# The last up-projection product of two tiles on the upper and lower 64 rows of TensorE, and the second network in pairs of tiles

## What is computed

```python
# 1: causal mixing over 7 tokens, weights = softmax of weight_gen per head (8 heads of 24)
out = einsum("bshk,bskhg->bshg", softmax(weight_gen), windows_of_7(x))
# 2: gated network, d_ff 1536
xn = x / sqrt(mean(x * x) + 1e-6) * rms_g
y = (silu(xn @ w_gate) * (xn @ w_val)) @ w_out
# 3: second network, d_ff 2048
h = y @ w_in
out = (h * sigmoid(1.702 * h)) @ w_out2
```

## Time and profile before

| | |
|---|---|
| three runs, median (lowest, highest) | 1329.49 us (1329.16 to 1329.7) |
| profiled execution, span from first to last instruction | 1328.2 us |
| PE busy, share of the span | 1283.0 us, 97% |
| PE weight loads | 1088.3 us, 82% |
| DVE busy | 782.2 us, 59% |
| ACT busy | 679.0 us, 51% |
| POOL busy | 101.7 us, 8% |

### The profile page before, as it was taken

The page is one execution under the profiler, slowest core; times in us unless marked ns, Lnnn a source line. Parts: engine busy times, 40 slices in busy tenths (PEclk is TensorE's granted clock), DMA queues, the critical chain, the costliest instruction groups (busy, mean ns, idle before and its releaser), DMA issues.

```text
span 1328.2 us, 19585 instructions
## 1 busy us (share of the span) xinstructions
PE 1283.0 (97%) x6304; PEld 1088.3 (82%) x6304; DVE 782.2 (59%) x1186; ACT 679.0 (51%) x1194; POOL 101.7 (8%) x104
## 2 busy tenths in 40 slices
PE   0889999999999999999999999999999999999998
PEld 0667888889888888888889888888888889888898
DVE  5889475473846638475473846638475473843432
ACT  2343646555464553646555454553645555464454
POOL 6873000000000000000000000000000000000000
PEclk9999999999999999999999999999999999999999
DMA  5331000000100001000000100001000000000000
GB/s 141 87 108 39 1 16 31 16 31 4 41 0 15 30 3 41 0 15 30 15 30 3 41 0 15 30 3 41 0 15 30 15 30 0 12 0 13 1 13 13
DMA packets 14525, 32.21 MB, mean 24 GB/s; under 512 B 1828, under 2 KB 7842, under 8 KB 14496
## 3 DMA queue, kind: packets, MB, share of 16 engines
q1 hardware_dynamic: 14496, 31.85, 7.6%
HBM read 25.55 MB, written 6.29 MB: 24 GB/s over the span
## 4 chain that ended last, share of the span: by engine, by line
PE 92%; DVE 1%; issue 1%; ACT 0%; DVEq 0%
PE acc L754 15%; PE up_ps L706 11%; PE up_ps L713 11%; PE up_ps L714 11%; PE up_ps L707 11%; PE up_ps L710 11%; PE acc L755 7%; PE acc L734 3%; PE acc L731 3%; PE acc L735 3%; PE acc L732 3%; PE acc L733 3%; PE acc L768 0%; DVE hidden L654 0%; PE acc L772 0%
## 5 line engine op out<-in xcount | busy, mean ns | idle before, releaser
L669 DVE TENSOR_TENSOR h_lo<-hidden,h_hi 128x512 fp32r<-128x512 f32 x448 | 315.7, 706 | 382.0 <-ACT h_hi L487 381.5
L487 ACT CAST h_hi<-hidden 128x512 fp32r<-128x512 f32 x448 | 278.7, 622 | 186.1 <-DVE hidden L654 178.5
L754 PE MATMUL acc<-out_w,h_hi 128*128 128x384 f32 x1024 | 306.4, 355 | 0.0
L755 PE MATMUL acc<-out_w,h_lo 128*128 128x192 f32 x1024 | 257.6, 252 | 0.0
L471 ACT ACTIVATE hidden<-up_ps 128x512 f32<-128x512 f32 x256 | 153.2, 598 | 203.2 <-PE up_ps L714 202.9
L466 ACT ACTIVATE silu<-up_ps 128x512 f32<-128x512 f32 x192 | 114.5, 596 | 196.1 <-PE up_ps L714 195.7
L654 DVE TENSOR_TENSOR hidden<-silu,up_ps 128x512 f32<-128x512 f32 x192 | 131.8, 687 | 129.0 <-ACT silu L466 128.8
L755 PEld LDWEIGHTS acc<-out_w,h_lo 128*128 128x128 f32 x1024 | 195.0, 190 | 10.2
L754 PEld LDWEIGHTS acc<-out_w,h_hi 128*128 128x128 f32 x1024 | 192.2, 188 | 10.6
L706 PE MATMUL up_ps<-x_hi,up_w 128*128 128x512 f32 x384 | 154.5, 402 | 3.1 <-DVE hidden L654 2.0
L713 PE MATMUL up_ps<-x_rest,up_w 128*128 128x512 f32 x384 | 152.7, 398 | 3.8 <-DVE x_rest L593 3.8
(11 more groups left out here) (80 smaller groups left out, 1671.1 us busy)
## 6 DMA issues: line engine op xcount, KB each, us to landing
x_win<-in_x_dram SPq DMA_DIRECT2D x14, 960.0 KB
out_dram<-out_sb SPq DMA_DIRECT2D x15, 384.0 KB, 2.3
stage<-in_moe_w_out_dram SPq DMA_DIRECT2D x13, 192.0 KB, 2.5
logits<-in_weight_gen_dram SPq DMA_DIRECT2D x16, 112.0 KB, 2.0
stage<-in_moe_w_in_dram SPq DMA_DIRECT2D x4, 256.0 KB, 2.9
stage<-in_moe_w_in_dram SPq DMA_DIRECT2D x8, 128.0 KB, 2.9
stage<-in_moe_w_val_dram SPq DMA_DIRECT2D x3, 256.0 KB, 4.2
stage<-in_moe_w_val_dram SPq DMA_DIRECT2D x6, 128.0 KB, 2.8
```

Source lines behind the costliest of these rows:

```text
L487: nc.scalar.copy(h_hi[:, u % 4, :], hidden[:, u % 2, :]).then_inc(hi_ready, 1)
L669: nc.vector.tensor_tensor(h_lo[:, u % 4, :], hidden[:, u % 2, :], h_hi[:, u % 4, :].bitcast(F32), ALU.subtract).then_inc(lo_ready, 1)
L754: nc.tensor.matmul(acc[:, j, 0:2 * D], h_hi[:, n % 4, tile], w, start=n == 0, stop=False)
L755: ins = nc.tensor.matmul(acc[:, j, 0:D], h_lo[:, n % 4, tile], w[:, 0:D], start=False, stop=n == U2 - 1)
```

## The change

`up` becomes `up_full`, which makes the first four of the five products, and `up_halves`, which makes the fifth for two tiles with two products of 64 rows each: the first tile's on rows 0 to 63 of the array, with `x_rest` (hi part), the second tile's on rows 64 to 127, with a copy of the same hi part there, `x_twin` (or `y_twin`). The built program gives the first four a tile of 128x128 at position (0, 0) and the two others tiles of 64x128 at positions (0, 0) and (64, 0). The product of the weights' lo part with the activations' lo part is no longer in the sum. The weights' lo parts move from `up_w[:, :, 3, :]` to `pair_lo`, where rows 0 to 63 belong to a pair's first tile and rows 64 to 127 to its second. A pair is gate and value tile of a unit, or tiles n and n+1 (n even) of the second network. That network is therefore done in pairs of tiles: PE makes both, then two `down2`. `down2(n-2)` and `down2(n-1)` now follow the pair n, and two of them, behind u = 0, are left for the next block. DVE makes the twin copy between the two operations of `split_rest`. POOL waits for its own preceding chunk ahead of each one, and subtracts the rest of `w_in` in two pieces of 64 rows.

```diff
-        up_w = sb("up_w", [P, 2 * U1 + U2, 4, P], F32R)
+        up_w = sb("up_w", [P, 2 * U1 + U2, 3, P], F32R)
+        pair_lo = sb("pair_lo", [P, PAIRS, P], F32R)
...
+        x_twin, y_twin = sb("x_twin", [P, N], F32R), sb("y_twin", [P, N], F32R)
...
             def split_chunk(n, hi_here):
...
+                if n:
+                    pool.wait_ge(chunk_split, n)
...
-                for hi, lo, f in parts:
+                for a, (_, _, lo, f, hi) in enumerate(parts):
+                    if a and kind == "rest":
+                        pool.wait_ge(even_split, even_splits(n))
                     last = nc.gpsimd.tensor_tensor(lo, f, hi.bitcast(F32), ALU.subtract)
...
-            def split_rest(g, f32, rest, hi_sem, ready):
+            def split_rest(g, f32, rest, twin, hi_sem, ready):
                 nc.vector.tensor_copy(rest[0:REST, :], f32[0:REST, 1, :]).then_inc(hi_sem, 1)
+                nc.vector.tensor_copy(twin[REST:P, :], f32[0:REST, 1, :])
                 dve.wait_ge(hi_sem, g * 2 + 2)
                 nc.vector.tensor_tensor(rest[REST:P, :], f32[0:REST, 1, :], rest[0:REST, :].bitcast(F32),
                                         ALU.subtract).then_inc(ready, 1)
...
-            def up(ps, t, hi, lo, rest, hi_sem=None, ready=None, g=None):
+            def up_full(ps, t, hi, lo, rest, hi_sem=None, ready=None, g=None):
...
                 nc.tensor.matmul(ps[:, :], w[:, 2, :], rest[:, :], start=False, stop=False)
-                return nc.tensor.matmul(ps[:, :], w[:, 3, :], rest[:, :], start=False, stop=True)
+
+            def up_halves(ps_a, ps_b, pair, rest, twin):
+                a = nc.tensor.matmul(ps_a[:, :], pair_lo[0:REST, pair, :], rest[0:REST, :], start=False, stop=True)
+                b = nc.tensor.matmul(ps_b[:, :], pair_lo[REST:P, pair, :], twin[REST:P, :], start=False, stop=True)
+                return a, b
...
-                        up(pair[1], U1 + u, x_hi, x_lo, x_rest).then_inc(up_done, 1)
-                    else:
+                        up_full(pair[1], U1 + u, x_hi, x_lo, x_rest)
+                        _, val = up_halves(pair[0], pair[1], u, x_rest, x_twin)
+                        val.then_inc(up_done, 1)
+                    elif u % 2 == 0:
...
-                            pe.wait_ge(gelu_done, i * U2 + (n - 3 - U2))
+                            pe.wait_ge(gelu_done, i * U2 + (n - 2 - U2))
...
+                        up_full(pair[1], 2 * U1 + n + 1, y_hi, y_lo, y_rest)
+                        even, odd = up_halves(pair[0], pair[1], U1 + n // 2, y_rest, y_twin)
+                        even.then_inc(up_done, 1)
+                        odd.then_inc(up_done, 1)
                     if u == 0 and not (is_block(i, 0) or is_block(i, 1)):
-                        down2(i - 1, U2 - 3)
                         down2(i - 1, U2 - 2)
-                    if u == 1 and not (is_block(i, 0) or is_block(i, 1)):
                         down2(i - 1, U2 - 1)
...
-                    if u >= U1 + 3:
-                        down2(i, u - U1 - 3)
+                    if u >= U1 + 2 and u % 2 == 0:
+                        down2(i, u - U1 - 2)
+                        down2(i, u - U1 - 1)
```

More of the change, by code:

```diff
@@ L121, in staged_count, with even_splits @@
         return sum(32 if chunks[q][1] == "rest" else 16 for q in range(c + 1) if place_of(q) == place_of(c))
+    def even_splits(n):
+        return sum(chunks[q][0] is w_in and chunks[q][1] == "rest" for q in range(n + 1))
     def chunks_for_up(m, gated):
@@ L351, in split_chunk @@
                 parts = split_parts(src, kind, t)
+                if n:
+                    pool.wait_ge(chunk_split, n)
                 if hi_here:
                     pool.wait_ge(staged[place_of(n)], staged_count(n))
-                    for hi, _, f in parts:
-                        last = nc.gpsimd.tensor_copy(hi, f)
+                    for hi, f, _, _, _ in parts:
+                        if hi is not None:
+                            last = nc.gpsimd.tensor_copy(hi, f)
                     last.then_inc(chunk_hi, 1)
                 pool.wait_ge(chunk_hi, n + 1)
-                for hi, lo, f in parts:
+                for a, (_, _, lo, f, hi) in enumerate(parts):
+                    if a and kind == "rest":
+                        pool.wait_ge(even_split, even_splits(n))
                     last = nc.gpsimd.tensor_tensor(lo, f, hi.bitcast(F32), ALU.subtract)
+                    if a == 0 and kind == "rest" and len(parts) > 1:
+                        last.then_inc(even_split, 1)
                 last.then_inc(chunk_split, 1)
@@ L389, in _ @@
                 split_chunk(n, True)
+            pool.wait_ge(chunk_split, len(chunks))
             with pool.Fori(2, GROUPS) as g:
@@ L399, in chunk_hi_half @@
                 act.wait_ge(staged[place_of(n)], staged_count(n))
-                for hi, _, f in split_parts(places[place_of(n)], kind, t):
-                    last = nc.scalar.copy(hi, f)
+                for hi, f, _, _, _ in split_parts(places[place_of(n)], kind, t):
+                    if hi is not None:
+                        last = nc.scalar.copy(hi, f)
                 last.then_inc(chunk_hi, 1)
@@ L602, in split_x @@
                 dve.wait_ge(x_scaled, g * 2 + 2)
-                split_rest(g, x_f32, x_rest, x_hi_ready, x_ready)
+                split_rest(g, x_f32, x_rest, x_twin, x_hi_ready, x_ready)
             def empty_y_rest(g, downs):
@@ L635, in split_y_rest @@
                 dve.wait_ge(rest_out, g + 1)
-                split_rest(g, y_f32, y_rest, y_hi_ready, y_ready)
+                split_rest(g, y_f32, y_rest, y_twin, y_hi_ready, y_ready)
             def run(i, slots, mixing):
@@ L777, in run @@
                 if is_block(i, GROUPS):
-                    for n in range(U2 - 3, U2):
+                    for n in range(U2 - 2, U2):
                         down2(i - 1, n)
@@ L826, in run @@
                         turn_x(i + 1)
-                    if slots[0] == 0 and 2 <= u < U1 + 2:
+                    if slots[0] == 0 and 2 <= u < U1:
                         down1(i, u - 2)
-                    if u >= U1 + 3:
-                        down2(i, u - U1 - 3)
+                    if slots[0] == 0 and u == U1:
+                        down1(i, U1 - 2)
+                        down1(i, U1 - 1)
+                    if u >= U1 + 2 and u % 2 == 0:
+                        down2(i, u - U1 - 2)
+                        down2(i, u - U1 - 1)
                 if is_block(i, 0):
```

42 lines of the change are left out of this document (29 added, 13 removed).

## The result

The changed kernel takes 1380.56 us (median of 4 runs, 1379.6 to 1381.02); beside it the kernel before took 1329.6 us (1329.16 to 1332.24). The ratio is 1.0376, 95% interval 1.0362 to 1.0391: **51 us slower**, where 1296.7 was forecast. It is above the range given.

The account below looks back on a forecast made before the run. PE was taken as the bound, except a DVE-bound start of about 114 us. Sum: 1328.2 - 36.2 + 1.5 + 1.2 + 0.7 = 1295.4, plus 1.3 from span to median: 1296.7 us; range 1262 to 1366.

Parts of the forecast that it names:

- the small terms: Additions outside the product pairs: twin copies in the start +1.5 and +1.2 us, the end +0.7, others zero; 3.4 us.
- The cost of changing the array: PE going from whole array to halves and back, 2 times a pair: taken as zero.
- The other bound given, 0.166 a change: At each array change, PE waits for the product before to end: 0.40 us record less 0.234 slot.
- The stagger of 0.11 between the halves: Second half's weights load when the first half starts, so a pair takes one slot + 0.11 us; 36.2 us saved.
- the 24 pairs of the start: Pairs in the two units of work before 114 us, in the DVE-bound stretch: counted as nothing.
- the 0.7 predicted: At the kernel's end, no next pair covers the second network's evicting chain before h_lo: +0.7 us.
- Emptying out_sb at zero: Moving unit 1's last down2 out shortens cover for emptying output accumulators: zero, 0.15 us slack; about 4 us if it fails.
- A stop at each change: At each pair's two seams PE lets the running product end first: 1362 us, or 1394 with staggered halves; chance 0.30.
- "half-hidden" stop: Partly hidden drain at the pair's seams, 0.05 to 0.08 us a change: 1290 to 1330 us; half of 0.30.
- No overlap: The two 64-row products of a pair follow one another, no slots saved or added: 1333 us; chance 0.10.
- At once: Both halves' weights load during the whole-array product before and both start together: 1264 us; chance 0.20.
- Either one 0.15 or more longer is the stop: Sign on PE's timeline: L751 to L755 beyond 0.23 us, or L755 to next whole product beyond 0.34.

Follow-up runs that it names:

- e2: Changed kernel with both 64-row products of a pair on the upper rows, so they can't run at once; 1456.3 us.
- e3: Changed kernel with each half product directly behind its own tile's four whole products, 4 array changes a pair instead of 2; 1573.26 us.
- e4: Changed kernel with only the upper half product of each pair made, the other left out; 1379.33 us.
- e1: Changed kernel with everything kept, but each pair's two last products made on all 128 rows, with no array change; 1334.3 us.
- e6: Changed kernel with both networks in fours: two gated units, or four tiles, share one stay in half mode; 1346.69 us.
- e5: Changed kernel with the first network's last products on the whole array, and the second network making four tiles, then four half products in one stay; 1334.47 us.
- e8: e5 with tiles 0 to 3 of each group back on the whole array, one at a time; three stays a group remain; 1329.67 us.
- e7: Changed kernel with the two halves first of a pair in the second network, in 6 of 8 pairs behind a 192-column product; 1379.23 us.

## Why the prediction was wrong

**What bounds the kernel: right.** PE before and after, with no starved stretch and the full clock in the loop. In the start the clock did not stay full (see the small terms).

**The cost of changing the array: this step failed.** "The trace has no price for going from the whole array to halves and back ... I take zero, because PE passes here between products of 512, 384, 192 and 128 columns with no gap beyond the weight load." That was evidence from changes of another kind. Measured: 0.32 us from the product's start to the next load behind 512 columns, 0.09 beyond the slot, and 0.11 us of load uncovered; 0.20 a change, 0.38 to 0.39 a stay in e2 and e3. By this term alone 296 pairs are 296 x 0.39 = 115 us worse than written. The other bound given, 0.166 a change, was near, but by two errors that partly cancel: it waited for the recorded end of the product, 0.40 us, where the load starts after 0.32, and it forgot that this load can then hide behind nothing.

**The stagger of 0.11 between the halves: wrong too,** in the other direction. L755 and L756 both start at 627.03, and their loads at 627.02 and 627.03. "In every row a load starts no earlier than the product before it" holds on one set of rows, not across two. The saving was therefore a whole slot a pair, 68.8 us and not 36.2. The Trainium skill, "TensorE: Matmul & The Clock Gate", Part 3, has products on different row groups start about 4 ns apart; the trace agrees, within its 0.01 us, and the 0.09 us a group that e4 gains by leaving the second one out, 0.005 us a pair, is of that size.

Put together anew: 296 x 0.385 - 68.8 is +45 us; the 24 pairs of the start, which I counted at nothing, would be 24 x 0.155 = 3.7; the small terms about 4. That is 53 us for the 51 measured; part of the start's pairs lies in waits that were there anyway.

**The small terms: near in sum, partly by luck.** I had +3.4 us; e1 has +4 (its interval is 2.9 to 5.4). The parts: the twin copy in the start was costed at 1.5 us, but from the x_rest copy's start to PE's first use it was 3.21 us before and is 3.54 now, since the subtraction behind it fell from 1.64 to 0.68 us. The same step of the changed kernel:

```profile
34.77 1.48 DVE L626 CAST x_rest<-x_f 64x512 fp32r<-64x512 f32 x1
36.28 1.38 DVE L628 CAST x_twin<-x_f 64x512 fp32r<-64x512 f32 x1
37.58 0.68 DVE L630 TENSOR_TENSOR x_rest<-x_f,x_rest 64x512 fp32r<-64x512 f32 x1
```

PE's longest wait for x_rest is 2.6 us, not 3.8. The second twin copy, ahead of group 1, was costed at 1.2 us. It made PE's wait for x_rest only 0.63 us longer, but the clock, for which the sum had no term, then fell. Before and changed, the product that waited, and the stretch from 92 to 94 us (columns as in the earlier trace rows):

```profile
91.54 0.50 PE L713 MATMUL up_ps<-x_rest,up_w 128*128 128x512 f32 x1 [1.55 <-DVE x_rest L593]
...
92.00:94.00 2.00, 2.00 (x11) 1.59 (x10) 0.89 (x2) 0.81 (x2) 1.92 (x3) 1.00 0.35 97
```

```profile
91.87 0.80 PE L751 MATMUL up_ps<-x_rest,up_w 128*128 128x512 f32 x1 [2.18 <-DVE x_rest L630]
...
92.00:94.00 2.00, 2.00 (x5) 1.36 (x5) 1.22 (x2) 0.29 (x1) 1.86 (x3) 0.50 0.29 97
```

The granted clock is 0.50 here, the lower of its two levels (1.2 of 2.4 GHz), and 5 products start where 11 did. The page's row of nines does not show so short a fall. In e1, which has the same fall, the eight products from 93.33 us take 3.50 us where the eight from 91.54 took 1.98 before: 1.5 us of e1's 4. Every run with the twin copy in the start has a fall between 90 and 106 us (in e6, with another order, it comes ahead of that wait); before, e5 and e8, without the copy and with a wait of 1.5 us for x_rest, stay at 1.00 there. No run takes away the copy alone, so that it brings on the fall is argued and not shown. What else makes up e1's start was not tried. At the end, from the last up-projection product's start to the last product's, there were 4.76 us (1319.81 to 1324.57) and are now 5.42 (1369.76 to 1375.18): +0.66 for the 0.7 predicted. Emptying out_sb at zero held: e1's group is 0.06 us above that of before. DVE's cover held: PE waited for `hidden` 0.9 us in all.

**The rivals.** "A stop at each change" is what happened: its place (both seams), its sign and its full form with the halves together, 1362 us. It was low by 0.03 us a change, 18 us in all. The Trainium skill, "TensorEngine Tiling (Array Packing)", Key Properties, says that changing the tiling mode drains the TensorE. The trace agrees: the load waits about 0.10 us behind the last column (e7), and once it is exposed it costs as much again. I gave this rival 0.30 and turned half of that into a "half-hidden" stop; a drain that must end before a load may start can't be hidden behind that load. The chances don't follow from the rivals either: with that half put between 1290 and 1330, faster would have been near 0.7 and slower 0.25, not 0.60 and 0.34. "No overlap" (1333) is refuted by e2 against the changed kernel. "At once" was right about the halves, and wrong only in having no stop.

**What the list of signs was good for.** "Either one 0.15 or more longer is the stop" missed narrowly as written: L751 to L755 shows 0.33 for 0.23 in the records. With the load that the record starts with, it is 0.44. The plainest sign was the gated unit: 3.67 us from one pair of halves to the next (623.36 to 627.03), neither 3.40 nor the old 3.51. Starts of records across a hidden and a bare load can't be subtracted as they stand.

## What to carry to other kernels

A stay on part of the array costs about 0.39 us here, whatever is done in it, against 0.23 for each 512-column slot that it saves; two half products save one slot and lose 0.155, four save two and gain about 0.06 (0.04 to 0.08 by the comparison taken). No kernel here with halves was faster than the kernel before by more than the noise. So collect half products until a stay saves at least two slots, and first see that there are banks for that many open sums and evicting engines with time for them, since a batch of tiles that end together starves the next batch (e5, e6). When a change brings in a state of an engine that no row shows, zero is not the nearest bound: price the seam with everything that it uncovers, above all the weight load. And a wait in the load queue is worth its length less the load's slack (0.17 us here), not its length.

## What the runs showed of the hardware

- Two products of 64 rows on the upper and the lower half of the array, 512 columns each, take the time of one: leaving the second out gains 0.09 us a group of 20 pairs (e4).
- At a change of the array the next load starts about 0.10 us after the last column went in: 0.18 us from start to next load behind 192 columns, 0.32 behind 512 (e7, after).
- Inside the halves loads are hidden again, on the same rows (e2: loads at 700.29 and 700.40) and on both (e6: 624.86 and 625.20, no stop). Only the change is dear.
- The cost stands on both sides: to the halves and back to the whole array take 0.31 to 0.32 us from the running product's start to the next load (after: 626.70 to 627.02; halves streaming from 627.14, next load at 627.45).
- The granted clock was 0.50 in the changed kernel from 92 to 94 us, after PE had stood 2.18 us for x_rest; it was 1.00 in the kernel before, after a wait of 1.55 us.
